# One decayed query, a compact state, and a score mask that moves from VectorE to GpSimd

## The reference

```python
f = 1.0 / (1.0 + np.exp(-f_logit))                 # B, H, S, D = 4, 8, 768, 48
for t in range(S):                                 # gated linear attention
    state = f[:, :, t, :, None] * state + np.einsum('bhd,bhe->bhde', k[:, :, t], v[:, :, t])
    y[:, :, t] = np.einsum('bhd,bhde->bhe', q[:, :, t], state)
x = y as 3072 tokens x 384
h = x @ w_in                                       # 384 x 2048
x = (h * tanh(softplus(h))) @ w_out                # 2048 x 384
out = (sigmoid(x @ w_gate) * (x @ w_val)) @ w_out2 # 384 x 1536, 1536 x 384
```

## Time and profile before

| what | value |
|---|---|
| runs | median 1061.21 us (1059.1 to 1064.91, 3 runs) |
| profiled execution | 1059.6 us, span of the profile 1057.6 us |
| attention stage (to the first MLP matmul) | 0 to 189.6 us of the span |
| TensorE busy | 1015.0 us, 96% |
| VectorE, ScalarE, GpSimd busy | 552.2, 541.1, 132.3 us |

### The profile page before, as it was taken

One profiled execution on the slowest core, in us unless ns is written; L12 is line 12 of the kernel. 1 busy time (PEld: TensorE's weight loads), 2 busy tenths in 40 slices (PEclk: granted clock), 3 DMA queues, 4 the chain that ended last, 5 costly groups with the idle time before them and its releaser, 6 DMA issues.

```text
span 1057.6 us, 14107 instructions
## 1 busy us (share of the span) xinstructions
PE 1015.0 (96%) x4765; PEld 824.8 (78%) x4765; DVE 552.2 (52%) x843; ACT 541.1 (51%) x969; POOL 132.3 (13%) x147
## 2 busy tenths in 40 slices
PE   4999999899999999999999899999999999999997
PEld 3777777688887888878888688888888888888885
DVE  6999998566667666667777622222222222222221
ACT  5677776577777777787777622121321122321212
POOL 2222212500000000004455420000000000000000
PEclk9999999899999999999999999999999999999999
DMA  5444442200000000001111100000100000100001
GB/s 149 143 140 132 140 138 78 60 1 1 1 1 1 0 0 0 0 0 43 48 45 46 46 22 2 0 1 1 60 0 0 0 0 0 60 0 1 1 1 60
DMA packets 35339, 37.54 MB, mean 35 GB/s; under 512 B 4064, under 2 KB 26080, under 8 KB 35296
## 3 DMA queue, kind: packets, MB, share of 16 engines
q1 hardware_dynamic: 35296, 36.98, 11.7%
HBM read 32.24 MB, written 4.72 MB: 35 GB/s over the span
## 4 chain that ended last, share of the span: by engine, by line
PE 81%; DVE 10%; issue 5%; ACT 3%; DVEq 0%; DMA 0%; SPq 0%; ACTq 0%
PE bank L841 26%; PE bank L843 26%; PE bank L842 26%; DVE prefix L576 2%; DVE probs L603 1%; ACT qt L412 1%; DVE suffix L578 1%; DVE state L620 1%; DVE xlo L627 1%; PE bank L784 1%; PE bank L761 1%; DVE state L614 1%; DVE kb L592 1%; DVE qb L589 1%; PE bank L779 1%
## 5 line engine op out<-in xcount | busy, mean ns | idle before, releaser
L841 PE MATMUL bank<-xhi,whi 128*128 (+1 forms) x720 | 285.0, 396 | 4.2 <-DVE xlo L721 2.6
L843 PE MATMUL bank<-xhi,wlo 128*128 (+1 forms) x720 | 283.7, 394 | 0.0
L842 PE MATMUL bank<-xlo,whi 128*128 (+1 forms) x720 | 281.0, 390 | 0.0
L841 PE MATMUL bank<-ghi,whi 128*128 128x512 f32 x504 | 200.4, 398 | 8.1 <-DVE glo L713 7.8
L741 DVE TENSOR_TENSOR prod<-prod,bank 128x512 f32<-128x512 f32 x72 | 49.5, 688 | 290.2 <-PE bank L843 290.2
L843 PE MATMUL bank<-ghi,wlo 128*128 128x512 f32 x504 | 198.2, 393 | 0.0
L842 PE MATMUL bank<-glo,whi 128*128 128x512 f32 x504 | 197.0, 391 | 0.0
L841 PEld LDWEIGHTS bank<-xhi,whi 128*128 128x128 f32 x720 | 135.5, 188 | 33.6 <-DVE xlo L721 3.0
L843 PEld LDWEIGHTS bank<-xhi,wlo 128*128 128x128 f32 x720 | 135.4, 188 | 32.3
L842 PEld LDWEIGHTS bank<-xlo,whi 128*128 128x128 f32 x720 | 135.7, 188 | 31.0
L521 ACT ACTIVATE prod<-bank 128x512 f32<-128x512 f32 x72 | 43.2, 600 | 188.0 <-PE bank L843 188.0
(11 more groups left out here) (70 smaller groups left out, 1060.3 us busy)
## 6 DMA issues: line engine op xcount, KB each, us to landing
raw<-w_out_dram SPq DMA_DIRECT2D x28, 192.0 KB, 2.4
xb<-f_dram SPq DMA_DIRECT2D x48, 96.0 KB, 2.4
kb<-k_dram SPq DMA_DIRECT2D x48, 96.0 KB, 2.2
qb<-q_dram SPq DMA_DIRECT2D x48, 96.0 KB, 2.2
vb<-v_dram SPq DMA_DIRECT2D x24, 192.0 KB, 2.4
out_dram<-rows_out SPq DMA_DIRECT2D x18, 256.0 KB, 2.2
raw<-w_in_dram SPq DMA_DIRECT2D x16, 192.0 KB, 2.6
raw<-w_gate_dram SPq DMA_DIRECT2D x12, 192.0 KB, 2.5
```

The costliest lines, as they stand in the source:

```text
L841: pe.matmul(ps, hi, xh, start=first, stop=False)
L842: pe.matmul(ps, hi, xl, start=False, stop=False)
L843: return pe.matmul(ps, lo, xh, start=False, stop=last)
```

## The change

The query is decayed once: the suffix scan runs first and has one more column, whose value is the chunk's total; its reciprocal seeds the prefix scan, so that `qb` itself is the query divided by the total. `qt`, `rtotal` and `q_scaled` go. The state has 48 columns per pair instead of 96 (each head on its own 64 rows), is multiplied by the total before it is used, and is not cleared between batches. Scores, state products and kᵀv are issued per head instead of per pair, with operands on half of the rows. ScalarE copies the scores of all heads from PSUM to `probs`, and GpSimd masks them there in place with one affine_select, after it has split the step's weight unit. The rows of w_in are stored in another order, since y's heads now lie even ones first.

```diff
 # SP queue, loads(b, n)
-                    wait(sp, f_done, g + 1)
+                    wait(sp, gates_done, g + 1)
...
-                    wait(sp, inter_done, g - 3)
+                    wait(sp, y_done, g - 3)
                     load_q(g + 2, n + 2)
                 if not isinstance(g, int) or g + 1 < B * NCH:
-                    wait(sp, ds_done, g - 1)
+                    if n == 1:
+                        wait(sp, y_done, g - 1)
+                    else:
+                        wait(sp, ds_done, (b if n > 1 else b - 1) * (NCH - 1) + (n - 2) % NCH + 1)
                     load_v(g + 1, n + 1)
                 load_unit(b, n)
 # GpSimd
-            run_a(pool, 0, 0, split_unit)
+            def high_unit(b, n):
...
+                pool.wait_ge(raw_in[s], (b * (NCH // STAGES) + n // STAGES + 1) * 16)
+                pool.tensor_copy(whi[:, bass.ds(unit, 1), :].squeeze(1), raw[:, s, :]).then_inc(w_hi_done, 1)
...
+            def mask(b, n):
+
+                pool.affine_select(out=probs[:, n % 2], in_=probs[:, n % 2], compare_op=ALU.is_ge, fill=0.0, base=0,
+                                   pattern=[[0, H], [1, C]], channel_multiplier=-1).then_inc(probs_done, 1)
+
+            def masks_and_weights(b, n):
+                unit, chunk = lag_a(b, n, 0), lag_a(b, n, 1)
+                if unit:
+                    high_unit(*unit)
+                if chunk:
+                    pool.wait_ge(copied_done, chunk[0] * NCH + chunk[1] + 1)
+                if unit:
+                    low_unit(*unit)
+                if chunk:
+                    mask(*chunk)
+
+            run_a(pool, 1, 1, masks_and_weights)
 # ScalarE
-                for a in range(PAIRS):
-                    for par in range(2):
-                        rows = slice(par * HALF, (par + 1) * HALF)
-                        ins = act.activation(qt[rows, a, par, :], qb[rows, n % NCH, a, :], ACT.Copy, scale=rtotal[rows, n % 2, a:a + 1])
-                    ins.then_inc(qt_done, 1)
+            def scores_copied(b, n):
+
+                g = b * NCH + n
+                wait(act, y_done, g - 1)
+                act.wait_ge(scores_done, g + 1)
+                act.activation(probs[:, n % 2], s_ps, ACT.Copy).then_inc(copied_done, 1)
...
-                for lag, do in ((0, gates), (2, k_rows), (4, x_high), (1, q_scaled), (3, y_rows)):
+                for lag, do in ((0, gates), (1, keep_total), (4, x_high), (2, k_rows), (3, y_rows), (1, scores_copied)):
 # VectorE
-                for half in range(2):
-                    dve.tensor_tensor(probs[:, n % 2, 4 * half:4 * half + 4, :],
-                                      s_ps[half][:, :].rearrange("p (h t) -> p h t", h=4),
-                                      causal[:, :].unsqueeze(1).to_broadcast([P, 4, C]), ALU.mult).then_inc(probs_done, 1)
...
+                    dve.tensor_tensor(state[:, :, :], state[:, :, :], ds_ps, ALU.add).then_inc(state_done, 1)
...
-                for lag, do in ((0, scans), (1, mask), (0, decay), (3, x_low), (2, carry)):
+                for lag, do in ((0, suffixes), (3, carry), (2, decay), (4, x_low), (0, k_decayed), (0, prefixes), (0, q_decayed)):
 # TensorE, scores and values
-                    pe.wait_ge(qt_done, PAIRS * g + a + 1)
-                    mm = pe.matmul(s_ps[a // 2][:, (a % 2) * 2 * C:(a % 2 + 1) * 2 * C], kb[:, n % 3, a, :],
-                                   qt[:, a, :, :].rearrange("p h t -> p (h t)"), start=True, stop=True)
+                    for par in range(2):
+                        rows = slice(par * HALF, par * HALF + D)
+                        mm = pe.matmul(s_ps[:, par * PAIRS + a, :], kb[rows, n % 3, a, :], qb[rows, n % NCH, a, :], start=True, stop=True)
...
-                pe.wait_ge(state_done, 2 * g + 1)
                 wait(pe, ysb_done, g)
-                pe.wait_ge(probs_done, 2 * g + 2)
+                pe.wait_ge(probs_done, g + 1)
...
+                if n > 0:
+                    pe.wait_ge(decay_done, b * (NCH - 1) + n)
+                    for a in range(PAIRS):
+                        for par in range(2):
+                            hd, rows = 2 * a + par, slice(par * HALF, par * HALF + D)
+                            mm = pe.matmul(y_ps[:, par, a * D:(a + 1) * D], qb[rows, n % NCH, a, :], state[rows, a, :],
+                                           start=False, stop=a == PAIRS - 1, skip_group_check=True)
...
+                for a in range(PAIRS):
+                    for par in range(2):
+                        hd, rows = 2 * a + par, slice(par * HALF, (par + 1) * HALF)
+                        mm = pe.matmul(ds_ps[rows, a, :], kt_sb[:, n % 2, a, rows], vb[:, n % 3, hd * D:(hd + 1) * D], start=True, stop=True)
                 mm.then_inc(ds_done, 1)
```

More of the change, by code:

```diff
@@ L558, in _ @@
             dve.memset(consts[:, 2:3], -Y_SHIFT).then_inc(zeroed, 1)
-            dve.memset(state[:, :, :], 0.0).then_inc(state_done, 1)
             dve.wait_ge(zeroed, ZEROED - 3)
@@ L574, in scans @@
                 dve.wait_ge(gates_done, g + 1)
-                wait(dve, qdec_done, g)
-                dve.tensor_tensor_scan(flat(prefix), gate[:, 0:PAIRS * C], flat(first), 0.0, ALU.mult, ALU.add).then_inc(prefix_done, 1)
-                wait(dve, kdec_done, g)
-                dve.tensor_tensor_scan(flat(suffix)[:, ::-1], gate[:, 1:PAIRS * C + 1][:, ::-1], flat(last)[:, ::-1],
-                                       0.0, ALU.mult, ALU.add).then_inc(suffix_done, 1)
-            def decay(b, n):
+                wait(dve, kdec_done, g)
@@ new lines, in suffixes, with k_decayed @@
+                wait(dve, total_done, g)
+                wait(dve, first_done, g)
+                dve.tensor_tensor_scan(flat(suffix)[:, ::-1], gate[:, 1:PAIRS * (C + 1) + 1][:, ::-1], flat(last)[:, ::-1],
+                                       0.0, ALU.mult, ALU.add).then_inc(suffix_done, 1)
+            def k_decayed(b, n):
+                g = b * NCH + n
+                dve.wait_ge(suffix_done, g + 1)
+                wait(dve, prefix_done, g)
+                dve.reciprocal(first[:, :, 0], suffix[:, :, 0]).then_inc(first_done, 1)
+                dve.wait_ge(k_in[n % 3], (b * (NCH // 3) + n // 3 + 1) * 32)
+                dve.tensor_tensor(kb[:, n % 3], kb[:, n % 3], suffix[:, :, 1:C + 1], ALU.mult).then_inc(kdec_done, 1)
@@ L583, in decay, with prefixes, q_decayed @@
+            def prefixes(b, n):
+                g = b * NCH + n
+                dve.wait_ge(first_done, g + 1)
+                wait(dve, qdec_done, g)
+                dve.tensor_tensor_scan(flat(prefix), gate[:, 0:PAIRS * (C + 1)], flat(first), 0.0, ALU.mult, ALU.add).then_inc(prefix_done, 1)
+            def q_decayed(b, n):
                 g = b * NCH + n
+                dve.wait_ge(q_in[n % NCH], (b + 1) * 32)
                 dve.wait_ge(prefix_done, g + 1)
-                dve.tensor_scalar(out=total(g), in0=prefix[:, :, C - 1], scalar1=1.0, scalar2=None, op0=ALU.mult).then_inc(total_done, 1)
@@ L586, in decay @@
[L586 to L592 removed]
+                dve.tensor_tensor(qb[:, n % NCH], qb[:, n % NCH], prefix[:, :, 1:C + 1], ALU.mult).then_inc(qdec_done, 1)
@@ L607, in carry @@
[L607 to L621 removed]
+            def carry(b, n):
+                if n == NCH - 1:
+                    return
+                dve.wait_ge(ds_done, b * (NCH - 1) + n + 1)
+                if n == 0:
+                    dve.tensor_copy(state[:, :, :], ds_ps).then_inc(state_done, 1)
+                else:
+                    dve.tensor_tensor(state[:, :, :], state[:, :, :], ds_ps, ALU.add).then_inc(state_done, 1)
@@ L623, in x_low, with decay @@
+            def decay(b, n):
+                if n == 0:
+                    return
+                g = b * NCH + n
+                dve.wait_ge(total_done, g + 1)
+                dve.wait_ge(state_done, b * (NCH - 1) + n)
+                dve.tensor_tensor(state[:, :, :], state[:, :, :], total(g).unsqueeze(2).to_broadcast([P, PAIRS, D]), ALU.mult).then_inc(decay_done, 1)
             def x_low(b, n):
```

137 lines of the change are left out of this document (50 added, 87 removed).

## The result

The changed kernel takes 1202.74 us (median of 4 runs, 1200.81 to 1204.03) against 1061.81 us before: ratio 1.1325, 95% interval 1.1289 to 1.136. That is 141 us slower; forecast were 109 us (1170 us, range 1115 to 1212).

The account below looks back on a forecast made before the run. Attention was to be paced by a loop per chunk through weight transfer, GpSimd's split and mask, and TensorE; its terms sum to 12.35 us, ending attention 109.6 us later: 1170 us, range 1115 to 1212.

Parts of the forecast that it names:

- The loop: In attention, each chunk's mask waits through GpSimd's split and the weight transfer for an earlier kᵀv: 12.35 us a chunk.
- the drain: End of attention after the last kᵀv: values and state product in a row behind y's transposes, about 7.8 us.
- the forecast's own band: The main forecast's range: loop of 11.2 to 13.6 us, kernel 1145 to 1200 us, chance 0.52.
- kᵀv to cast: From the end of kᵀv(i-2) through SP's load and transfer to GpSimd's cast: 3.4 us (3.2 to 3.6).
- hand-over: Semaphore to TensorE between the end of GpSimd's mask and the values: 0.1 us a chunk.
- the slower clock: TensorE's half clock after idling, priced as one dip in four chunks: 0.4 us a chunk (0 to 2.2).
- rival 2: Clock falls in each chunk, mask or kᵀv at upper ends: loop 13.7 to 15 us, 1200 to 1228 us; chance 0.17.
- Contention: GpSimd's subtraction and mask and VectorE's two-SBUF-input operations exclude each other: 1.2 us a chunk (0 to 1.5).
- Rival 3: Weight transfer hidden before kᵀv(i-2), loop open, TensorE sets a 6.7 us period: about 1045 us; chance 0.03.
- What the profile was to show: GpSimd's cast waits for weights, values wait 4 to 6 us for the mask, SP's kᵀv wait longest, MLP 868 us.
- rival 1: All open terms cheap, clock held: loop 9.2 to 11.2 us, its sum starting at 3.24; 1102 to 1145 us; chance 0.26.

Follow-up runs that it names:

- experiment 1: Changed kernel with the SP queue issuing the weight unit's load before its wait for kᵀv of chunk i-2: 1082.87 us, 1.0211 of the kernel before.
- experiment 2: Changed kernel with GpSimd masking chunk i-1 before it splits weight unit i, transfer still late: 1082.18 us, 1.0213 of the kernel before.
- experiment 3: Changed kernel with one more 384-column subtraction on GpSimd in each step: 1220.47 us, 17.7 us more than the changed kernel.
- experiment 7: Kernel before, with only the scores issued per head (48 rows, 128 columns): 1119.67 us, 1.054 of the kernel before.
- experiment 4: Changed kernel with four unread 512-column matmuls a chunk before TensorE's wait for the mask: 1164.52 us, 1.0984 of the kernel before.
- experiment 6: The kernel of experiment 5 with one unread 512-column matmul ahead of the transposes of y: 1102.37 us, 1.0418 of the kernel before.
- experiment 9: The kernel of experiment 1 with unread matmuls ahead of y's transposes: one of 512 columns 1044.26 us; one of 512 and one of 256 columns 1049.56 us.
- experiment 5: Changed kernel with the mask back on VectorE, multiplying scores from PSUM, and ScalarE's copy gone: 1157.34 us, 1.0905 of the kernel before.

## Why the prediction was right, and which term was off

**The loop.** Direction, place and the loop itself were as forecast: kᵀv(i-2), transfer, split, mask(i-1), values, state product, kᵀv(i-1), once per chunk. It is shown by two separate cuts (experiments 1 and 2, 120 us each) and by the slope (experiment 3). The start came 1.3 us later than forecast (27.7 for 26.4), the 22 periods took 294.3 instead of 265.0 us, the drain 10.5 instead of 7.8, so attention ended 33 us later than the 299.2 forecast. The total lies in the stated range, but above the forecast's own band (1145 to 1200 us, chance 0.52).

**The sum of the loop, term by term,** for the period shown above (13.94 us for 12.35):

| term | forecast | measured |
|---|---|---|
| kᵀv to cast | 3.4 | 3.54 |
| cast, subtraction, mask, contention | 4.31 | 3.78 (159.16 - 155.38) |
| hand-over | 0.1 | 0.10 |
| values, state product, kᵀv, with the clock | 4.54 | 6.52 |

**The term that was mis-sized is the slower clock: 0.4 us forecast.** What the same matmuls take at full pace is in experiment 1's TensorE timeline:

```profile
77.94 1.98 PE L799 MATMUL banks<-vb,probs 128*128 128x48 f32 x16
79.85 1.09 PE L806 MATMUL banks<-state,qb 48*128 48x48 f32 x16
80.87 0.67 PE L816 MATMUL banks<-vb,kt_sb 128*64 128x48 f32 x16
81.47 1.16 PE L781 MATMUL banks<-qb,kb 48*128 48x128 f32 x16
```

1.91 + 1.02 + 0.67 = 3.6 us, so the clock costs 6.52 - 3.6 = 2.9 us a chunk, 2.5 more than forecast, 55 us in 22 periods. I had priced a dip now and then; half speed throughout was in the prediction as a bound (4.0) and as rival 2, and the result lies just inside rival 2's 1200 to 1228. The total stayed in the range partly by luck: in the period shown, terms that were too high took off about 1.1 us of the 2.5. My reason for weighing the clock low was wrong, and my cause was at best half of it: I looked at idle time alone. Experiment 1 (busy throughout, 0.50) and experiment 7 (no new wait, half pace) show that per-head scores on 48 rows keep the clock down without it; the state products, on 48 rows too, were not tried alone. In experiments 4, 6 and 9 a few whole-array matmuls bring part or most of it back. Whether the 48 rows count, or that two heads on different rows run at once, no run separates.

**Smaller terms.** The values took 1.91 us at full pace for the 1.74 forecast. The others were too high. The mask took 1.09 us undisturbed for the 1.45 estimated. The state product at full pace took 1.02 for the 1.3 taken between 0.87 and 1.74: 0.1175 us a record in the kernel after, while the values in the same chunk need 0.222, and the records start in pairs, 162.808 and 162.815 us, so the two heads of a pair overlap. By the Trainium skill's rule (TensorEngine Tiling (Array Packing), Key Properties: different tiles work in parallel), the trace agrees. Kᵀv's records start in pairs too; its 0.60 us from start to start still lies above the 0.47 that the prediction worked out for it.

**Contention** was forecast at 1.2 us. By GpSimd's means over the periods, the subtraction took 1.50 us instead of 1.00 (1.58 in the 17 of experiment 3's row, 1.24 in 5 more), the mask 1.35 instead of 1.09, and the cast 0.15 more than its undisturbed 0.50: 0.9 us. In the period shown, the subtraction began at 156.41 while the suffix scan ran to 157.33, and ended 0.78 us after it. By the Trainium skill (SBUF — State Buffer, Who interferes with whom), a VectorE instruction with two SBUF inputs and a GpSimd instruction that reads SBUF keep each other out; this row fits it, as the earlier trace rows did. No run takes this contention away by itself, so its 0.9 us is read, not tested.

**The rivals.** Rival 3 (transfer hidden) is what experiment 1 builds; it was priced at 1045 us for full clock. Experiment 1 came out 38 us above that. With the extra matmul it is met (1044.26), in part by luck, since that run also holds 0.85 us of work a chunk that the price did not have. What the profile was to show: the cast's wait for the transfer, SP's wait for kᵀv (161.9 us in 18 waits in the whole span) and the MLP's time are as written; the wait of the values for the mask is there but mostly stands under "issue", and the periods of 12.4 to 15 us reach outside the 11.2 to 13.6 allowed for right terms. (Two small readings in the prediction are off and change nothing: the last kᵀv before ends at 183.14, not 183.05 us, and rival 1's 3.24 stands in no row, where the shortest is 3.21.)

## What to carry to other kernels

An idle engine that runs a background job is not free for work on the path: whatever its next instruction waits for, here a weight transfer issued behind the end of an earlier chunk, becomes a wait of the path. Follow the new work's engine and its queue one step back before giving it the work, and issue the background transfer a step early or put the foreground work first (either was worth 120 us here). Cutting matmuls to part of the rows can cost the clock of the whole stage, so read the pitch of unchanged matmuls beside the change, and, where it has doubled, try one whole-array matmul a chunk.

## What the runs showed of the hardware

- TensorE busy 10.00 of 10 us, in stretch after stretch, was granted 0.50 while it ran 48-row scores and state products; the kernel before kept 1.00 at 94% busy with 128-row ones. Per-head scores alone did it (1060.28 to 1119.67 us); kᵀv per head, 64 output rows each, alone did not (1058.54 us).
- With per-head scores the clock fell after pauses of 0.34 to 1.33 us (experiments 1 and 7) and also without one (experiment 2), where the kernel before idled 9.4 us in its periods and kept it.
- One unread 512-column matmul of 0.85 us in each chunk took 39 us off experiment 1.
- Masking 128 x 1024 float32 with an affine_select on GpSimd took 1.09 us undisturbed, 1.35 us on average among VectorE's scans.
- The clock column of the profile reads 1.00 until the first recorded change; in ten of the thirteen traces (all but the kernel before, experiment 4 and kᵀv alone) matmuls before it ran at half pace. After the change, 16 records of the first values, at 23.01 us, took 3.58 us; experiments 5 and 7 ran at half pace to 280 and to 144 us.
